# Reordering ScalarE's and VectorE's queues in a fused mLSTM and two-layer gated MLP kernel

## The chip, the core and the metric

One core of a Trainium2 chip runs the whole kernel in one launch. The metric is device time in microseconds of that core. The engines are TensorE (PE in the profile, its weight loads PEld), VectorE (DVE), ScalarE (ACT), GpSimd (POOL) and SyncE (SP), which here only issues DMAs. Each engine executes its own list of instructions in order; semaphores are the only link between them.

## The reference

```
for t in range(768):                       # B=2, H=8, D=40: a stabilised mLSTM
    m_new  = max(f[t] + m, i[t])
    C = exp(f[t]+m-m_new) * C + exp(i[t]-m_new) * outer(v[t], k[t])
    n = exp(f[t]+m-m_new) * n + exp(i[t]-m_new) * k[t]
    y[t] = sigmoid(o[t]) * (C @ q[t]) / max(|n . q[t]|, 1)
x = y as [1536 tokens, 320]
x = (sigmoid(x @ w_gate) * (x @ w_val)) @ w_out          # layer 1, d_ff = 1536
xn = x / rms(x) * rms_g                                  # layer 2
g = xn @ w_gate2;  out = (g * sigmoid(g) * (xn @ w_val2)) @ w_out2
```

All data are float32. The kernel computes each product of two float32 operands from rounded parts: a high part (`_hi`) and the remainder (`_lo`), three matmuls in place of one.

## The kernel before, in words

The 1536 tokens are 12 tiles of 128 (`NT`), numbered alternately over the two batches. The mLSTM is done by tiles; its pieces have one-letter names that every engine's `piece` function knows: D (decay weights by a matmul, then Exp on ACT), S (q·k scores on PE, sigmoid of the output gate on ACT), N, K, I (numerator, state update, state read), R (decays of a group of tiles: small PE matmuls, then two small Exp on ACT), Y (division on DVE), T (three PE transposes of a finished tile, ACT copies them to `x_hi`, DVE writes the remainder `x_lo`).

The first layer takes two phases. Tiles 0 to 7 go through it in four blocks of two tiles (`NB0`): a block is twelve slots `hidden(k, f)`, each of 16 matmuls for one 128-wide slice f of the gate and value products, followed by four halves of `project`, the down projection. The lists in `WEAVE` put the mLSTM pieces of later tiles between these slots, in the same order on all engines. Then come the wide blocks (`NB1`, four of them, k = 0 to 3): k = 0 is layer 1 for tiles 8 to 11, k = 1 to 3 are layer 2 for all twelve tiles, four tiles at a time.

In a wide block `hidden_pair(k, i)`, i = 0 to 5, computes slices f = 2i and 2i+1 in four phases: own half of slice f, own half of f+1, other half of f, other half of f+1. So slice f is finished (`g_done`, `v_done`) at the end of the third phase and slice f+1 at the end of the fourth. Behind each slice n runs a chain on two engines: `sigmoid(n)` on ACT (L620), `gate(n)` on DVE (L853; in layer 2 L851 ahead of it), `h_high(n)` on ACT (a Copy, L626), `h_low(n)` on DVE (L857), which counts up `h_done`. PSUM has eight banks, four in use by a pair and four by the pair before, so two places in PE's list wait for this chain:

```
if i > 1:
    pe.wait_ge(h_done, n - 3)                 # hidden_pair, phase of slice n
...
pe.wait_ge(h_done, n0 + NF - 2 if wide(n0) else ...)   # project, at each first half
```

The first asks for the same slice of the pair two before; the second asks for ten of the twelve slices of the block before the down projection starts; within the first token tile each further slice is waited for by itself.

The weights are loaded raw by SP into three rotating buffers, rounded by ACT in `high(layer, c)` (twelve chunks a layer; c below 8 are gate and value weights, L533), and the remainder is made by POOL in `split(layer, c)` (L435, L440), in order of c. `hidden(0, f)` waits at f = 0, 3, 6, 9 for two more splits each. SP reloads a raw buffer when its split is done.

At the start ACT's list is: D of tiles 0 and 1, `high(0,0)`, sigmoids S of tiles 0 and 1, `high(0,1)`, `high(0,2)`, the fill of `d_lhs` (L607), T(0), T(1), D(2), `high(0,3)`, D(3), R(1); then the slots. PE's is: T(0), idle matmuls, T(1), D(2), D(3), `hidden(0,0)`, R(1), `hidden(0,1)`. ACT holds one set of function tables; the compiler puts an ACT_TABLE_LOAD ahead of an Exp that follows a Sigmoid and ahead of a Sigmoid that follows an Exp. Copies run under either set.

Of the kernel before, what the change touches and what calls it, by code (L numbers as in the profile page):

```python
# [4 lines left out]
F32 = mybir.dt.float32  # L5
# [3 lines left out]
ACT = mybir.ActivationFunctionType  # L9
# [4 lines left out]
P = 128  # L14
# [8 lines left out]
NF = FF // P  # L23
# [15 lines left out]
F1 = NB0 * NF  # L39
# [33 lines left out]
def mlstm_moe_kernel(nc, gates, qk_t, vok, w_gv, w_o, rms_g, out):  # L73
# [5 lines left out]
    with ctx:  # L79
        def sb(name, shape, dt):  # L80
            return ctx.enter_context(nc.sbuf_tensor(name, shape, dt))
# [60 lines left out]
        meansq = sb("meansq", [P, B], F32)  # L142
        rstd = sb("rstd", [P, B], F32)
        half_neg = sb("half_neg", [P, 1], F32)
        eps = sb("eps", [P, 1], F32)


# [15 lines left out]
        def wide(n):  # L163
            return n >= F1
# [23 lines left out]
        def exp_base(n):  # L188

            return 0 if n == 3 else base(n)  # L190
# [18 lines left out]
        def raw_of(lay, c):  # L209
            r = (raw0, raw1)[lay][c % 3]  # L210
            if c < GVC:
                return r.rearrange("p (k c) -> p k c", k=3)
            return r[:, 0:FC * DM].rearrange("p (k c) -> p k c", k=FC)
# [34 lines left out]
        def part_of(j):  # L248
            return [j0 <= j < j1 for j0, j1 in PARTS].index(True)
# [272 lines left out]
        def _(act):  # L522
            def high(lay, c):
                whi = (whi0, whi1)[lay]
                if lay == 0:
                    act.wait_ge(raw0_in[c % len(raw0)], 16 * (c // len(raw0) + 1))
                else:
                    act.wait_ge(raw1_in[c % len(raw1)], 16 * (c // len(raw1) + 1))
                if c < GVC:
                    if lay == 1:  # L530
                        act.wait_ge(g_done, F1 + FC * (c // 2 + 1))
                        act.wait_ge(v_done, F1 + FC * (c // 2 + 1))
                    act.activation(wgv_hi[:, c, :, :], raw_of(lay, c), ACT.Copy).then_inc(whi, 1)  # L533
                else:
                    if lay == 1:
                        act.wait_ge(o_done, NT)
                    f0 = (c - GVC) * FC
                    act.activation(wo_hi[:, f0:f0 + FC, :], raw_of(lay, c), ACT.Copy).then_inc(whi, 1)

            def piece(what):  # L540
                kind, n, *_ = what
                b = n % B
                if kind == "D":
                    for i in range(2):
                        act.wait_ge(d_done, 2 * n + i + 1)
                        if n >= B and i == 0:
                            act.wait_ge(n_done, n - B + 1)
                        act.activation(wexp[b][:, 4 * i:4 * i + 4, :],
                                       bank[exp_base(n) + i][:, :].rearrange("p (q t) -> p q t", t=P),
                                       ACT.Exp).then_inc(e_done, 1)  # L550
                    if n < NT - B:

                        if n >= B:
                            act.wait_ge(vk_done, n - B + 1)
                        act.wait_ge(e_done, 2 * n + 2)
                        act.activation(el[:, b, :], wexp[b][:, :, P - 1], ACT.Copy).then_inc(el_done, 1)
                elif kind == "F":

                    act.wait_ge(rows_done, part_of(n) + 1)
                    act.wait_ge(fill_done, 2)  # L560
                    if n > 1:
                        act.wait_ge(d_done, 4 * n)
                    for w in range(2):
                        act.dma_start(d_rhs[R + w:R + w + 1, :, :].bitcast(F32),
                                      l_row[Q * w:Q * w + R, n % LR * P:(n % LR + 1) * P].bitcast(F32)).then_inc(flat_in, 16)
                elif kind == "R":
                    j0, j1 = PARTS[n]
                    act.wait_ge(r_mm, n)
                    act.activation(ecol[:, j0:j1, :], decay_t[:, j0:j1, :], ACT.Exp)
                    act.activation(gcol[:, j0:j1, :, :], decay_end[:, j0:j1, :, :], ACT.Exp).then_inc(r_exp, 1)  # L570
                elif kind == "S":
                    act.wait_ge(vo_in[b], 16 * (n // B + 1))
                    act.activation(o_sig[b], o_sig[b], ACT.Sigmoid).then_inc(osig_done, 1)
                elif kind == "T":
                    act.wait_ge(t_done, n + 1)
                    if n == 4:
                        act.wait_ge(split0, WCH)
                    if n == 8:
                        act.wait_ge(rows_done, len(PARTS))
                    act.activation(x_hi[:, n, :, :], t_view(bank[base(n) + 2]), ACT.Copy).then_inc(xh_done, 1)  # L580
                elif kind == "O":
                    act.wait_ge(ot_done, n + 1)
                    act.activation(x_hi[:, n, :, :], t_view(o_bank(n)), ACT.Copy).then_inc(xh2_done, 1)

            act.wait_ge(consts, 1)
            for b in range(B):
# [20 lines left out]
            act.activation(d_lhs[HALF:P, :, :, :], hide[HALF:P, :, :].unsqueeze(1).to_broadcast([HALF, NJ - 1, 2, P]),  # L607
                           ACT.Copy).then_inc(fill_done, 1)
            piece(("T", 0))
            piece(("T", 1))  # L610
            piece(("D", 2))
            high(0, 3)
            piece(("D", 3))
            piece(("R", 1))

            def sigmoid(n):
                act.wait_ge(g_done if wide(n) else v_done, n + 1)
# [4 lines left out]
            def h_high(n):  # L622
                act.wait_ge(hf_done, n + 1)
                if n % NF == 0 and n:
                    act.wait_ge(o_done, M0 + T1 * ((n - F1) // NF) if wide(n) else B * (n // NF))
                act.activation(h_view(n, 0), v_view(n), ACT.Copy).then_inc(hhi_done, 1)  # L626
# [21 lines left out]
            for k in range(NB1):  # L648
                for f in range(NF):
                    n = F1 + NF * k + f  # L650
                    sigmoid(n)
                    if f % 2:
                        h_high(n - 1)
                        h_high(n)
                    if k == 0 and f % FC == FC - 1:
                        high(1, 2 * (f // FC))
                        high(1, 2 * (f // FC) + 1)
                for t in range(T1):
                    m = M0 + T1 * k + t
                    if k == 0 and t < T1 - 1:  # L660
                        square(m)
                        piece(("O", M0 - B + t))
                        continue
                    if k == 0:
                        piece(("O", M0 - B + t))
                        square(m)
                        continue
                    act.wait_ge(o_done, m + 1)
                    if k == 1 and 0 < t <= B:
                        act.wait_ge(ot_done, NT - B + t)  # L670
                    if k > 1:
                        act.wait_ge(out_sent[t], 16 * (k - 1))
                    act.activation(y_out(t), o_view(m), ACT.Copy).then_inc(oe_done, 1)
                    if k == 1 and t < B:
                        piece(("O", NT - B + t))
                if k == 0:
                    for c in range(GVC, WCH):
                        high(1, c)
# [3 lines left out]
        def _(dve):  # L682
# [172 lines left out]
            def h_low(n):  # L855
                dve.wait_ge(hhi_done, n + 1)
                dve.tensor_tensor(h_view(n, 1), v_view(n), h_view(n, 0).bitcast(F32), ALU.subtract).then_inc(h_done, 1)  # L857
# [21 lines left out]
            for k in range(NB1):  # L879
                for f in range(NF):  # L880
                    n = F1 + NF * k + f
                    gate(n)
                    if f % 2:
                        h_low(n - 1)
                        h_low(n)
                if k == 0:
                    for t in range(T1):
                        piece(("O", M0 - B + t))
                        norm(M0 + t)
                elif k == 1:  # L890
                    for t in range(B):
                        piece(("O", NT - B + t))
# [3 lines left out]
        def _(pe):  # L896
# [242 lines left out]
            piece(("T", 1))  # L1139
            piece(("D", 2))  # L1140
            piece(("D", 3))
            hidden(0, 0)
            piece(("R", 1))
            for k in range(NB0):
                for slot in range(NF + 4):
                    if slot < NF:
                        if k or slot:
                            hidden(k, slot)
                    else:
                        t, half = divmod(slot - NF, 2)  # L1150
                        project(NF * k, B * k + t, t, half)
                    for what in WEAVE[k][slot]:
                        piece(what)
# [66 lines left out]
```

## Time and profile before

| | us |
|---|---|
| median of three runs (452.08 to 452.28) | 452.1 |
| the profiled execution's own time | 452.08 |
| its span, first to last instruction | 450.3 |
| PE busy | 444.9 (99%) |
| PEld busy | 404.2 (90%) |
| DVE busy | 211.3 (47%) |
| ACT busy | 186.8 (41%) |
| POOL busy | 97.0 (22%) |

Busy times are shares of the span. Matmuls overlap in the pipeline: a row of 128x512 in the wide blocks lasts 0.39 us while pairs of them start 0.23 us apart, so distances between starts, not durations, give TensorE's pace. In the timelines the first two columns are the start and the length in us; a bracket at the end holds the idle time of that engine ahead of the instruction, with what ended it.

### The profile page before, as it was taken

How to read it: one execution, taken by the hardware profiler on the slowest of the kernel's cores; microseconds unless marked ns; L12 is line 12 of the kernel's file. 1: busy time of each engine (PE TensorE's matmuls, PEld its weight loads, DVE VectorE, ACT ScalarE, POOL GpSimd, SP SyncE). 2: the span in 40 equal slices, each digit the busy share in tenths (PEclk: the TensorE clock that was granted, in tenths of full speed). 3: DMA queues.
4: the chain of work that ended last, by engine and by line, in shares of the span. 5: the costliest groups of instructions: out<-in, count | busy, mean ns of one | idle time of the engine just before them, and what ended most of it. 6: DMA issues, size and time to landing. Idle time of an engine off the chain costs nothing.

```text
span 450.3 us, 10548 instructions
## 1 busy us (share of the span) xinstructions
PE 444.9 (99%) x4489; PEld 404.2 (90%) x4489; DVE 211.3 (47%) x465; ACT 186.8 (41%) x355; POOL 97.0 (22%) x141
## 2 busy tenths in 40 slices
PE   8999999999999999999999999999999999999997
PEld 3799999999999999988889988889988899888897
DVE  8746746854476356424332217561055630256510
ACT  8976367554654463215544144231032320133310
POOL 2999711012101200013656172000000000000000
PEclk9999999999999999999999999999999999999999
DMA  7684600210221012100443110000000000000000
GB/s 253 208 264 136 206 3 1 77 62 17 75 75 58 22 45 90 70 1 2 121 132 102 44 45 1 1 0 31 31 2 0 1 16 29 16 1 2 0 31 29
DMA packets 10127, 25.91 MB, mean 58 GB/s; under 512 B 1376, under 2 KB 4480, under 8 KB 10080
## 3 DMA queue, kind: packets, MB, share of 16 engines
q1 hardware_dynamic: 9760, 25.15, 17.2%
q8 instruction: 35, 0.57, 0.5%
q10 hardware_dynamic: 320, 0.08, 0.1%
q14 instruction: 12, 0.10, 0.1%
HBM read 23.18 MB, written 1.97 MB: 56 GB/s over the span
## 4 chain that ended last, share of the span: by engine, by line
PE 95%; DVE 2%; POOL 2%; issue 0%; ACT 0%; POOLq 0%; DVEq 0%
PE bank L1097 36%; PE bank L1113 10%; PE bank L1115 9%; PE bank L1114 9%; PE bank L1046 8%; PE bank L1047 8%; PE bank L1049 5%; PE bank L965 2%; PE bank L996 2%; PE bank L899 2%; PE bank L984 1%; POOL wgv_lo L435 1%; PE bank L939 1%; PE bank L1005 1%; DVE first L832 1%; POOL wgv_hi L440 0%
## 5 line engine op out<-in xcount | busy, mean ns | idle before, releaser
L1097 PE MATMUL bank<-x_hi,wgv_hi 64*128 64x512 f32 x576 | 105.8, 388 | 0.0
L620 ACT ACTIVATE sg<-bank 128x256 f32<-128x256 f32 (+1 forms) x96 | 47.1, 492 | 131.0 <-PE bank L1097 82.3
L1097 PE MATMUL bank<-x_lo,wgv_hi 64*128 64x512 f32 x480 | 93.9, 386 | 0.0
L853 DVE TENSOR_TENSOR bank<-sg,bank 128x256 f32<-128x256 f32 (+1 forms) x96 | 53.8, 561 | 67.2 <-ACT sg L620 65.6
L1046 PE MATMUL bank<-x_hi,wgv_hi 128*128 128x256 f32 x288 | 80.5, 290 | 0.4 <-POOL wgv_hi L440 0.4
L1047 PE MATMUL bank<-x_lo,wgv_hi 128*128 128x256 f32 x288 | 78.3, 282 | 0.0
L1113 PE MATMUL bank<-wo_hi,h_hi 128*128 128x320 f32 x240 | 75.4, 314 | 0.0
L1097 PE MATMUL bank<-x_hi,wgv_lo 64*128 64x512 f32 x384 | 75.1, 386 | 0.0
L1115 PE MATMUL bank<-wo_hi,h_lo 128*128 128x320 f32 x240 | 74.1, 309 | 0.0
L1114 PE MATMUL bank<-wo_lo,h_hi 128*128 128x320 f32 x240 | 74.1, 309 | 0.0
L1097 PEld LDWEIGHTS bank<-x_hi,wgv_hi 64*128 64x128 f32 x576 | 54.4, 184 | 11.5 <-issue 0.7
L851 DVE TENSOR_TENSOR sg<-sg,bank 128x512 f32<-128x512 f32 x36 | 24.7, 687 | 83.0 <-ACT sg L620 83.0
L1046 PEld LDWEIGHTS bank<-x_hi,wgv_hi 128*128 128x128 f32 x288 | 55.0, 191 | 1.6 <-DVE x_lo L814 0.6
L1047 PEld LDWEIGHTS bank<-x_lo,wgv_hi 128*128 128x128 f32 x288 | 55.1, 191 | 0.0
L1049 PE MATMUL bank<-x_hi,wgv_lo 128*128 128x256 f32 x192 | 54.2, 283 | 0.0
L1097 PEld LDWEIGHTS bank<-x_lo,wgv_hi 64*128 64x128 f32 x480 | 45.4, 184 | 8.9
L1113 PEld LDWEIGHTS bank<-wo_hi,h_hi 128*128 128x128 f32 x240 | 45.1, 188 | 1.5 <-issue 1.4
L626 ACT ACTIVATE h_hi<-bank 128x256 fp32r<-128x256 f32 (+1 forms) x84 | 39.8, 474 | 15.0 <-DVE bank L853 15.0
L857 DVE TENSOR_TENSOR h_lo<-bank,h_hi 128x256 fp32r<-128x256 f32 (+1 forms) x84 | 44.8, 534 | 1.3
L1114 PEld LDWEIGHTS bank<-wo_lo,h_hi 128*128 128x128 f32 x240 | 45.1, 188 | 0.0
L1115 PEld LDWEIGHTS bank<-wo_hi,h_lo 128*128 128x128 f32 x240 | 45.1, 188 | 0.0
L1097 PEld LDWEIGHTS bank<-x_hi,wgv_lo 64*128 64x128 f32 x384 | 36.3, 184 | 7.3
(125 smaller groups left out, 546.8 us busy)
## 6 DMA issues: line engine op xcount, KB each, us to landing
step<-in_vok SPq DMA_DIRECT2D x12, 324.0 KB, 3.2
step<-in_qk_t SPq DMA_DIRECT2D x24, 160.0 KB
step<-in_w_gv SPq DMA_DIRECT2D x6, 576.0 KB, 3.9
raw_p<-in_w_gv SPq DMA_DIRECT2D x5, 576.0 KB, 3.9
raw_x<-in_w_gv SPq DMA_DIRECT2D x5, 576.0 KB, 5.0
step<-in_vok SPq DMA_DIRECT2D x10, 160.0 KB, 4.2
raw_x<-in_w_o SPq DMA_DIRECT2D x3, 480.0 KB, 3.5
raw_p<-in_w_o SPq DMA_DIRECT2D x3, 480.0 KB, 3.5
```

Source lines behind the costliest of these rows:

```text
L620: act.activation(sg_view(n), g_view(n), ACT.Sigmoid).then_inc(sg_done, 1)
L626: act.activation(h_view(n, 0), v_view(n), ACT.Copy).then_inc(hhi_done, 1)
L851: dve.tensor_tensor(sg_view(n), sg_view(n), g_view(n), ALU.mult).then_inc(silu_done, 1)
L853: dve.tensor_tensor(v_view(n), sg_view(n), v_view(n), ALU.mult).then_inc(hf_done, 1)
L857: dve.tensor_tensor(h_view(n, 1), v_view(n), h_view(n, 0).bitcast(F32), ALU.subtract).then_inc(h_done, 1)
L1046: pe.matmul(ps, wgv_hi[:, wc, s, cs], x_hi[:, xs, s, :], start=(s == 0), stop=False)
L1047: mm = pe.matmul(ps, wgv_hi[:, wc, s, cs], x_lo[:, xs, s, :], start=False, stop=(s == 2))
L1049: pe.matmul(ps, wgv_lo[:, wc, s, cs], x_hi[:, xs, s, :], start=False, stop=False)
L1097: mm = pe.matmul(ps(n), w, x, start=own and (s, p) == (0, 0), stop=last and not own)
L1113: pe.matmul(ps, h_view(n0 + f, 0)[:, ts], wo_hi[:, f, :], start=(f == 0), stop=False)
L1114: pe.matmul(ps, h_view(n0 + f, 0)[:, ts], wo_lo[:, f, :], start=False, stop=False)
L1115: mm = pe.matmul(ps, h_view(n0 + f, 1)[:, ts], wo_hi[:, f, :], start=False, stop=(f == NF - 1))
```

## The change

Four edits. (1) A one-column Exp into a new tile `spare` is put on ACT between T(0) and T(1). (2) `high(0,3)` goes from between D(2) and D(3) to behind R(1) on ACT. (3) On PE `hidden(0,0)` goes behind R(1). (4) In the wide blocks, `h_high(n-1)` on ACT and `h_low(n-1)` on DVE follow `sigmoid(n)` and `gate(n)` for every n, instead of two of them after every odd n; the last slice's follow the loop, on ACT in block k = 0 behind `high(1,6)` and `high(1,7)`.

```diff
+        spare = sb("spare", [P, 1], F32)
...
             piece(("T", 0))
+
+            act.activation(spare[:, :], half_neg[:, :], ACT.Exp)
             piece(("T", 1))
             piece(("D", 2))
-            high(0, 3)
             piece(("D", 3))
             piece(("R", 1))
+            high(0, 3)
...  (ScalarE, wide blocks)
                     sigmoid(n)
-                    if f % 2:
+                    if f:
                         h_high(n - 1)
-                        h_high(n)
                     if k == 0 and f % FC == FC - 1:
                         high(1, 2 * (f // FC))
                         high(1, 2 * (f // FC) + 1)
+                h_high(F1 + NF * k + NF - 1)
...  (VectorE, wide blocks)
                     gate(n)
-                    if f % 2:
+                    if f:
                         h_low(n - 1)
-                        h_low(n)
+                h_low(F1 + NF * k + NF - 1)
...  (TensorE, start)
             piece(("D", 3))
-            hidden(0, 0)
             piece(("R", 1))
             for k in range(NB0):
                 for slot in range(NF + 4):
                     if slot < NF:
-                        if k or slot:
-                            hidden(k, slot)
+                        hidden(k, slot)
```

## Rows read from the trace of the kernel before

**Rows 1.** The chain that ended last, by engine, from the page.
```profile
PE 95%; DVE 2%; POOL 2%; issue 0%; ACT 0%; POOLq 0%; DVEq 0%
```
**Rows 2.** Windows of wide block k=1: length, busy by engine, granted clock, DMA.
```profile
260.00:323.00 63.00, 63.00 (x512) 55.41 (x512) 26.45 (x41) 20.34 (x37) 11.15 (x14) 1.00 0.05 17
```
**Rows 3.** Timeline of PE, from D(3)'s matmuls to slot 3.
```profile
18.41 1.20 PE L939 MATMUL bank<-d_rhs,d_lhs 128*128 128x256 f32 x8
20.02 0.35 PE L1046 MATMUL bank<-x_hi,wgv_hi 128*128 128x256 f32 x1 [0.42 <-POOL wgv_hi L440]
...
21.89 0.28 PE L1047 MATMUL bank<-x_lo,wgv_hi 128*128 128x256 f32 x1
...
22.47 0.39 PE L1046 MATMUL bank<-x_hi,wgv_hi 128*128 128x256 f32 x1
22.70 0.28 PE L1047 MATMUL bank<-x_lo,wgv_hi 128*128 128x256 f32 x1
...
27.62 0.28 PE L1046 MATMUL bank<-x_hi,wgv_hi 128*128 128x256 f32 x1
```
**Rows 4.** Timeline of ACT from T(1) to R(1).
```profile
18.68 0.49 ACT L580 ACTIVATE x_hi<-bank 128x384 fp32r<-128x384 f32 x1 [0.39 <-PE bank L899]
19.20 1.28 ACT L548 ACT_TABLE_LOAD   x1
20.49 1.09 ACT L548 ACTIVATE tail<-bank 128x512 f32<-128x512 f32 x2
...
21.80 1.15 ACT L533 ACTIVATE wgv_hi<-raw_p 128x1152 fp32r<-128x1152 f32 x1
...
24.19 0.17 ACT L570 ACTIVATE gcol<-bank 128x8 f32<-128x8 f32 x1
```
**Rows 5.** Timeline of all engines, the DVE row of T(1).
```profile
19.21 0.56 DVE L814 TENSOR_TENSOR x_lo<-bank,x_hi 128x384 fp32r<-128x384 f32 x1 [0.32 <-ACT x_hi L580]
```
**Rows 6.** Timeline of POOL, the ends of split(0,1) and split(0,3).
```profile
18.87 1.00 POOL L440 TENSOR_TENSOR wgv_hi<-raw_x,wgv_hi 64x384 fp32r<-64x384 f32 x1
...
25.16 0.99 POOL L440 TENSOR_TENSOR wgv_hi<-raw_p,wgv_hi 64x384 fp32r<-64x384 f32 x1
```
**Rows 7.** Timeline of ACT, end of wide block k=0.
```profile
239.14 2.21 ACT L533 ACTIVATE wgv_hi<-step 128x1152 fp32r<-128x1152 f32 x2
```
**Rows 8.** Timeline of DVE, end of wide block k=0: gate(10).
```profile
236.32 0.70 DVE L853 TENSOR_TENSOR bank<-sg,bank 128x512 f32<-128x512 f32 x1 [2.15 <-ACT sg L620]
```
**Rows 9.** Timeline of PE, block k=0: first matmul of project, and its slice 10.
```profile
237.14 0.41 PE L1113 MATMUL bank<-wo_hi,h_hi 128*128 128x320 f32 x1
...
241.64 0.31 PE L1113 MATMUL bank<-wo_hi,d_rhs 128*128 128x320 f32 x1
```
**Rows 10.** Timeline of ACT, wide block k=1, slices 8 to 10.
```profile
292.53 0.60 ACT L620 ACTIVATE sg<-bank 128x512 f32<-128x512 f32 x1 [2.53 <-PE bank L1097]
...
294.61 0.60 ACT L626 ACTIVATE h_hi<-bank 128x512 fp32r<-128x512 f32 x1
...
299.33 0.60 ACT L620 ACTIVATE sg<-bank 128x512 f32<-128x512 f32 x1 [2.53 <-PE bank L1097]
```
**Rows 11.** Timeline of DVE, wide block k=1, slices 8 to 10.
```profile
295.47 0.69 DVE L853 TENSOR_TENSOR bank<-sg,bank 128x512 f32<-128x512 f32 x1
296.07 0.68 DVE L857 TENSOR_TENSOR h_lo<-bank,h_hi 128x512 fp32r<-128x512 f32 x1
...
299.96 0.69 DVE L851 TENSOR_TENSOR sg<-sg,bank 128x512 f32<-128x512 f32 x1 [2.44 <-ACT sg L620]
300.68 0.70 DVE L853 TENSOR_TENSOR bank<-sg,bank 128x512 f32<-128x512 f32 x1
```
**Rows 12.** Timeline of PE, the first matmul of project in block k=1.
```profile
300.77 0.41 PE L1113 MATMUL bank<-wo_hi,h_hi 128*128 128x320 f32 x1
```
**Rows 13.** Timeline of PE, idle matmuls at the start and later.
```profile
1.26 6.22 PE L1125 MATMUL bank<-inter 128*128 128x512 bf16 x21 [1.26 <-DVE inter L821]
...
15.70 1.04 PE L1125 MATMUL bank<-inter 128*128 128x512 bf16 x4
```

## The prediction, made before the changed kernel ran

> **What bounds the kernel now.** I read the chain of waits first. Nearly all of the chain that ended last is TensorE [rows 1], and in a window over a wide block TensorE is busy for all of its 63.00 us at a granted clock of 1.00 [rows 2]. So there is nothing later in the run that could take up a delay: whatever holds TensorE back at one place is added to the end, and whatever lets it start earlier is taken off. The other engines matter only where TensorE waits for them, or comes close to it. I then read the timelines of each engine around the four edits: 16 to 28 us for the first three, and the end of each wide block for the fourth.
>
> **Edits 1 and 3, the start.** TensorE ends D(3) at 18.41 + 1.20 = 19.61 and starts `hidden(0,0)` at 20.02 [rows 3]. It waits for two things that come close together: the second split, 18.87 + 1.00 = 19.87 [rows 6], and the remainder of tile 1, 19.21 + 0.56 = 19.77 [rows 5]. The idle 0.42 us is put down to the first, but the second has only 0.10 us of room.
>
> What edit 3 takes away: R(1) and the two switches around it. `hidden(0,0)` starts its last matmul at 21.89, and `hidden(0,1)` its second at 22.70 [rows 3]. Sixteen matmuls from 20.02 to 21.89 are 0.12 apart (1.87 / 15 = 0.125, with a longer first step). Without R(1) in between, the second of the next slot would start two steps after 21.89, at 22.13. That is 0.57 earlier. R(1) itself fits in the idle time: with its switches it takes under 22.47 - 21.89 = 0.58 [rows 3], and the gap is at least 0.41 and, as follows, becomes longer. It waits for nothing late: its inputs, the row ends on VectorE, are made before the scores of tiles 0 and 1.
>
> What edit 1 adds: ScalarE ran out of work at 18.68 - 0.39 = 18.29, then waited for T(1)'s transposes, copied them to 18.68 + 0.49 = 19.17, and only then loaded the Exp tables, 1.28 us [rows 4]. With the small Exp behind T(0) the load starts at 18.32, ends at 19.60, the Exp follows at 19.61 (the next activation starts 0.01 after a load: 19.20 + 1.28 to 20.49 [rows 4]) and takes 0.17 at most, a little less until the next one starts; I take 0.15. The copy of T(1) then starts at 19.76, not 18.68: 1.08 late. Only 0.39 us of the load is hidden in ScalarE's idle time, and the rest is put in front of a copy that TensorE needs. Its end moves to 20.25, the remainder's end on VectorE from 19.77 to 20.85, and `hidden(0,0)` starts some 0.05 later, at 20.90: 0.88 late. Edits 1 and 3 together: +0.88 - 0.57 = +0.31 us. From both sides: if the table load did not hold up the copy behind it, T(1) would be as early as now and the start would gain the whole 0.57; if R(1) filled nothing and the small Exp cost its full 0.17, the loss would be 0.90. I take +0.3, since the load's row leaves ScalarE no room for another instruction.
>
> The row has the load at 1.28 us and the Exp 0.01 behind it [rows 4]. The Trainium skill ("ScalarE: Activation LUTs", section "What ACT_TABLE_LOAD costs") gives a switch of sets 1.28 us and a drain of 1.38 beside it, 2.66 together. By that rule the copy of T(1) would be another 1.38 late and the start would cost +1.7, not +0.3. The row shows no such drain on either side of the load, so the trace does not agree here, and the sum goes by the row.
>
> **Edit 2, the first weights.** ScalarE is done with D(2), D(3) and R(1) sooner: `high(0,3)` was in between, from 21.80 for 1.15 [rows 4]. Now T(1)'s copy ends at 20.25 and D(2)'s Exps follow without a load, 0.3 earlier than 20.49. D(3) and R(1) then end at 24.36 - 1.15 - 0.3 = 22.9, and `high(0,3)` ends near 24.0 instead of 22.95. POOL's split(0,3) ended at 25.16 + 0.99 = 26.15 [rows 6] and now ends at about 27.2. TensorE asks for it in slot 3, at 27.62, now 27.9 [rows 3]. Room is left, 0.7 us, so it costs nothing. If ScalarE or POOL slipped by more than that, each further microsecond would be one for TensorE; the same delay, reduced by a short idle of POOL, goes through the later splits and raw loads, where slots 6 and 9 have more room than slot 3. I take 0, with 0 to +0.7.
>
> **Edit 4, the wide blocks.** This is the costly one. Now slice 9, the second of pair 4, is finished on the other engines right after pair 4, 6.8 us ahead of its use. In the new order `h_high(9)` stands behind `sigmoid(10)`, and `h_low(9)` behind `gate(10)`. Slice 10 is finished by TensorE only at the end of the third phase of pair 5; a single phase later TensorE reaches `project` and asks for ten slices, slice 9 among them.
>
> Block k = 1: `sigmoid(10)` starts at 299.33 [rows 10], L851 at 299.96 and L853 at 300.68 [rows 11]. The L857 behind an L853 starts 0.60 after it (295.47 to 296.07) and lasts 0.68 to 0.69. So `h_low(9)` runs from 301.28 to 301.97. `h_high(9)`, 0.60 long [rows 10], is done by 300.53 and is not in the way. TensorE's `project` begins at 300.77 now [rows 12] and at 301.97 + 0.05 = 302.02 then: a stall of 1.25 us. Blocks 2 and 3 have the same instructions at the same distances, so 3 x 1.25 = 3.75.
>
> Block k = 0 has no L851. `gate(10)` starts at 236.32 [rows 8], `h_low(9)` at 236.92, ending at 237.61; `project` moves from 237.14 [rows 9] to 237.66: 0.52 us.
>
> Is there a second loss inside the blocks? Phase two of pair i waits for the odd slice of pair i - 2, which now hangs on the even slice of pair i - 1. In k = 1 that is slice 7 behind slice 8: `sigmoid(8)` at 292.53 [rows 10], and the chain takes 301.97 - 299.33 = 2.64, so 295.17. TensorE starts the second phase of pair 5 later than that: pair 5 begins about when slice 9 is done, 1.6 us (a phase of 14 steps at 0.23 for two) behind slice 8, and its first phase of 16 matmuls lasts 1.8, so near 295.8. Room 0.6: nothing lost. In k = 0, `high(1,6)` and `high(1,7)`, 2.21 us for both [rows 7], now stand ahead of `h_high(11)`. `h_high(10)` starts near 237.8, the two run from 238.3 to 240.5, `h_high(11)` to 241.0, `h_low(11)` to 241.75. TensorE needs slice 11 one slice (three matmuls, 0.44) behind 241.64 [rows 9], plus the stall of 0.52, near 242.6. Room 0.8: nothing. If the raw chunk for `high(1,7)` came late, that room would be used first.
>
> **The sum.** +0.3 (start) + 0 (edit 2) + 0.52 (k = 0) + 3.75 (k = 1 to 3) = +4.6 us. The profiled execution took 452.08, which is the median of the runs within 0.02, so 456.7; I say 456.6, as the small Exp may overlap more.
>
> **The rivals.**
> (a) The covers of 0.6 to 0.8 us above are too thin: a split at slot 3, `h_low(7)` in the second phase, or `h_high(11)` is late. For it: three such places, each with under 1 us. Against it: all three are computed from rows that repeat within 0.01. It would give +0.5 to +1.5 more, about 457.7.
> (b) The clock falls in the new idle stretches ahead of `project`. At the start of the run, after an idle stretch of 1.26, TensorE needed 6.22 us for 21 matmuls of a kind that later run 1.04 for four, 0.22 apart; that is some 1.5 us more than 20 x 0.22 + 0.38 = 4.8 [rows 13]. If it fell in all three stretches of 1.25 us: +4.5 more, 461. Against it: the clock held 1.00 over idle 0.42 [rows 3], and the gaps stay short beside the busy time around them. The rule in the Trainium skill ("TensorE: Matmul & The Clock Gate", section "Part 1: The HAM clock gate") that an idle array falls back to 1.2 GHz speaks for it in kind.
> (c) Not slower: `h_done` of slice 9 comes before TensorE asks. That would need the chain sigmoid, gate, h_low behind slice 10 to be shorter than 300.77 - 299.33 = 1.44 us in k = 1, where the rows give 2.64; from that point on the stall is nothing, and only the start is left, +0.3 or, with the table load hidden too, -0.57. It would give 451.5 to 452.4, say 452.3. It could be so only if VectorE or ScalarE ran another order than the diff says.
>
> **How the numbers follow.** Forecast 0.82, (a) 0.09, (b) 0.05, (c) 0.04. The forecast's own range is from the start's bound without the late copy (-0.57, so 455.8) to 457.2. The range for 8 in 10 reaches some way to (a): 455.6 to 457.9. A difference of 0.2%, 0.9 us, is about what can be told from no change; slower by more than that holds for the forecast, (a) and (b), 0.95; (c) is within it, 0.04; faster 0.01.
>
> **What would show it.** The profile after should have four idle stretches of PE ahead of the down projection (L1113), 0.5 us once and 1.25 three times, released by VectorE's L857; `hidden(0,0)` starting at 20.9, released by VectorE's L814, with `hidden(0,1)` right behind; ACT_TABLE_LOAD at 18.3; no PE idle in slots 3 to 9 or in the second phases; clock 1.00. The forecast is wrong if the stretches ahead of L1113 are missing, or if PE idles anywhere else by more than 0.3 us.

## The result and the profile after

The changed kernel takes 456.8 us (median of four runs, 456.64 to 457.32) against 452.09: 4.7 us or 1.05% more, ratio 1.0105, interval 1.0088 to 1.0122. The forecast was 456.6 in 455.6 to 457.9. The profiled execution took 456.61 with a span of 454.8, 4.5 longer than before.

The page after, its busy times by engine, the granted clock and the chain by engine:

```profile
PE 445.1 (98%) x4489; PEld 404.1 (89%) x4489; DVE 208.1 (46%) x465; ACT 184.3 (41%) x356; POOL 96.5 (21%) x141
...
PEclk9999999999999999999999999999999999999999
...
PE 93%; DVE 3%; ACT 3%; issue 1%; ACTq 0%; DVEq 0%
```

TensorE works as long as before (445.1 against 444.9); the 4.5 us are time in which it waits. Where it waits, the groups of its instructions with the idle time ahead of them show at once (name, count, busy us and mean ns, idle us and releaser):

```profile
L1049 PE MATMUL bank<-x_hi,wgv_hi 128*128 128x256 f32 x288 | 80.4, 290 | 0.8 <-DVE x_lo L817 0.8
...
L1116 PE MATMUL bank<-wo_hi,h_hi 128*128 128x320 f32 x240 | 75.4, 314 | 4.0 <-DVE more_lo L860 4.0
```

The first is the start, the second the four first matmuls of `project`. L1116 and L860 are the L1113 and L857 of before. No other group waits more than it did. The same four places in the timeline of PEld, whose idle time also holds the switch between two kinds of matmul. Before, the rows at these places all read 0.35:

```profile
237.94 0.19 PEld L1116 LDWEIGHTS bank<-wo_hi,h_hi 128*128 128x128 f32 x1 [0.88 <-DVE more_lo L860]
...
302.82 0.19 PEld L1116 LDWEIGHTS bank<-wo_hi,h_hi 128*128 128x128 f32 x1 [1.60 <-DVE more_lo L860]
...
367.06 0.19 PEld L1116 LDWEIGHTS bank<-wo_hi,h_hi 128*128 128x128 f32 x1 [1.60 <-DVE more_lo L860]
...
430.64 0.19 PEld L1116 LDWEIGHTS bank<-wo_hi,h_hi 128*128 128x128 f32 x1 [1.59 <-DVE more_lo L860]
```

0.88 - 0.35 = 0.53, then 1.25, 1.25, 1.24: together 4.27. What stands behind them in block k = 1 is this piece of VectorE's timeline, to be laid beside [rows 11]:

```profile
300.75 0.69 DVE L854 TENSOR_TENSOR sg<-sg,bank 128x512 f32<-128x512 f32 x1 [2.87 <-ACT sg L623]
301.47 0.69 DVE L856 TENSOR_TENSOR bank<-sg,bank 128x512 f32<-128x512 f32 x1
302.08 0.68 DVE L860 TENSOR_TENSOR more_lo<-bank,d_rhs 128x512 fp32r<-128x512 f32 x1
```

The L860 at 302.08 is `h_low(9)`. It ends at 302.76, and TensorE starts at 302.82. VectorE had been idle for 2.87 us ahead of `gate(10)`, and ScalarE for 4.12 us ahead of `sigmoid(10)`: between them they had had the time to do `h_high(9)` and `h_low(9)`, but the order of both lists forbade it.

The start, TensorE's timeline first (to be read beside [rows 3]), then ScalarE's (beside [rows 4]):

```profile
18.41 1.19 PE L942 MATMUL bank<-d_rhs,d_lhs 128*128 128x256 f32 x8
19.53 0.23 PE L950 MATMUL bank<-ident,l_r 16*128 16x16 f32 x1
19.69 0.28 PE L953 MATMUL bank<-l_end,ones 16*64 16x8 f32 x4
20.82 0.38 PE L1049 MATMUL bank<-x_hi,wgv_hi 128*128 128x256 f32 x1 [0.84 <-DVE x_lo L817]
```

```profile
17.79 0.49 ACT L581 ACTIVATE x_hi<-bank 128x384 fp32r<-128x384 f32 x1
18.30 1.28 ACT L612 ACT_TABLE_LOAD   x1
19.60 0.20 ACT L612 ACTIVATE spare<-half_neg 128x1 f32<-128x1 f32 x1
19.71 0.47 ACT L581 ACTIVATE x_hi<-bank 128x384 fp32r<-128x384 f32 x1
```

R(1) is in the gap, the table load is in front of T(1)'s copy, and `hidden(0,0)` starts at 20.82, 0.80 late. Slot 3 starts at 27.89 against 27.62: 0.27 late, the shift that the start leaves. 4.27 + 0.27 = 4.54 is the whole of the 4.5.

### The profile page after: what moved, and what is told of

Its sections match the earlier page's. It is cut to its first block, busy times and chain, and to the rows that moved or that the text cites. A ratio compares the mean times of both kernels' runs of the same rounds, so it can differ in the third digit from the quotient of the medians.

```text
span 454.8 us, 10549 instructions
## 1 busy us (share of the span) xinstructions
PE 445.1 (98%) x4489; PEld 404.1 (89%) x4489; DVE 208.1 (46%) x465; ACT 184.3 (41%) x356; POOL 96.5 (21%) x141
## 4 chain that ended last, share of the span: by engine, by line
PE 93%; DVE 3%; ACT 3%; issue 1%; ACTq 0%; DVEq 0%
PE bank L1100 35%; PE bank L1116 10%; PE bank L1118 9%; PE bank L1117 9%; PE bank L1049 8%; PE bank L1050 8%; PE bank L1052 5%; PE bank L968 2%; PE bank L999 2%; PE bank L902 2%; PE bank L987 1%; PE bank L942 1%; PE bank L1008 1%; ACT wgv_hi L534 1%; DVE more_lo L860 1%
## 5 line engine op out<-in xcount | busy, mean ns | idle before, releaser
L1116 PE MATMUL bank<-wo_hi,h_hi 128*128 128x320 f32 x240 | 75.4, 314 | 4.0 <-DVE more_lo L860 4.0
L854 DVE TENSOR_TENSOR sg<-sg,bank 128x512 f32<-128x512 f32 x36 | 24.6, 683 | 88.7 <-ACT sg L623 88.7
L1116 PEld LDWEIGHTS bank<-wo_hi,h_hi 128*128 128x128 f32 x240 | 45.1, 188 | 5.8 <-DVE more_lo L860 5.7
L860 DVE TENSOR_TENSOR h_lo<-bank,h_hi 128x256 fp32r<-128x256 f32 (+1 forms) x84 | 44.6, 531 | 0.2
```

Of the source, the lines that this page charges most:

```text
L854: dve.tensor_tensor(sg_view(n), sg_view(n), g_view(n), ALU.mult).then_inc(silu_done, 1)
L1116: pe.matmul(ps, h_view(n0 + f, 0)[:, ts], wo_hi[:, f, :], start=(f == 0), stop=False)
```

## Experiments

Each time is a median over the runs of a comparison in which the kernel before took 452.08 to 452.11.

**order_only**, edit 4 alone: the two `if f % 2` loops replaced as in the change, nothing at the start.

> Edit 4 alone, on the kernel before. Theory (slice 9's h_low behind gate(10) makes TensorE wait ahead of project): idle 0.5 + 1.25 + 1.25 + 1.25 us of PE ahead of project and nowhere else, time 452.1 + 4.25 = 456.35. Rival (the loss needs the later start, or the start carries more than 0.3): under 455.5.

456.39 us (456.36 to 456.43), ratio 1.0094 (1.0080 to 1.0108). PE's idle time ahead of L1113 is 4.0 us in four places, as in the changed kernel. Edit 4 costs 4.3.

**start_only**, edits 1 to 3 alone.

> Edits 1 to 3 alone, wide blocks as before. Theory: hidden(0,0) 0.8 late, R(1) in the gap takes 0.57 off, so 452.1 + 0.3 = 452.4, and no PE idle after slot 0. Rival (the late weights of edit 2 cost something): over 452.8.

452.43 us (452.36 to 453.02), ratio 1.0009 (1.0000 to 1.0018): +0.34. The profiled execution, one of the slower ones (452.85), has no idle row of PE after the start. Together with order_only that is 4.6, against 4.7 for the whole change. The parts add up.

**pe_swap**, edit 3 alone.

```diff
-            hidden(0, 0)
             piece(("R", 1))
...
-                        if k or slot:
-                            hidden(k, slot)
+                        hidden(k, slot)
```

> Edit 3 alone: hidden(0,0) behind R(1) on TensorE, ScalarE's list as before. Theory: R(1) lies wholly in the idle time ahead of hidden(0,0), which still starts at 20.02; the time falls by 0.57 to 451.5. Rival (R(1) pushes hidden(0,0) back by its own length): 452.1, no change.

451.63 us (451.53 to 451.88), ratio 0.9990 (0.9981 to 0.9999): -0.47. In TensorE's timeline R(1) starts at 19.75 and `hidden(0,0)` at 20.13 with no idle time between:

```profile
18.64 1.19 PE L939 MATMUL bank<-d_rhs,d_lhs 128*128 128x256 f32 x8
19.75 0.23 PE L947 MATMUL bank<-ident,l_r 16*128 16x16 f32 x1
19.91 0.28 PE L950 MATMUL bank<-l_end,ones 16*64 16x8 f32 x4
20.13 0.39 PE L1046 MATMUL bank<-x_hi,wgv_hi 128*128 128x256 f32 x1
```

R(1) takes 0.38 with its switch and pushes `hidden(0,0)` back by 0.1 in this execution, in which D(2) was late as well (D(3)'s row starts at 18.64, not 18.41). The fastest of the eleven took 451.53, the time that the theory gives, and the rival's 452.1 is out. This is the only version here that is faster than before, by 0.1%, with an interval that just leaves out 1.

**warm_only**, edit 1 alone, the line with `act.activation(spare, ..., ACT.Exp)`.

> Edit 1 alone: the one-column Exp between T(0) and T(1). Theory: only the 0.4 us of ScalarE's idle time hide the table load, the copy of T(1) and so hidden(0,0) come 0.8 later: 452.9. Rival (the load runs beside the copy of T(1)): 452.1. With a drain of 1.38 us beside the load, as the Trainium skill, page ScalarE: Activation LUTs, section What ACT_TABLE_LOAD costs, has it, 454.3.

453.10 us (452.93 to 454.40), ratio 1.0026 (1.0015 to 1.0037): +1.0, where 0.8 was expected. In the profiled execution (452.96) `hidden(0,0)` starts at 20.84, 0.82 late, and PE idles 1.23 ahead of it, released by the DVE row of T(1); the rest of the 1.0 is the spread of the seven. The load is not beside the copy. A drain is not seen either: the median is 1.2 below 454.3, and in the rows of the changed kernel above the Exp follows the load's end (19.58) by 0.02. One of the seven took 454.40, but at a granted clock of 0.996, where the other six have 1.000; the last section comes back to it.

**nine_early**, the changed kernel with slice 9 alone in the old order.

```diff
-                    if f:
+                    if f and f != 10:
                         h_high(n - 1)
+                    if f == 9:
+                        h_high(n)
...  (and the same with h_low on VectorE)
```

> The changed kernel, but slice 9 of each wide block as before: h_high(9) and h_low(9) directly behind slice 9's own sigmoid and gate, all other slices in the new order. Theory (only slice 9 is late for TensorE): all four stalls vanish, 452.4, as edits 1 to 3 alone. Rival (the new order costs in the inner pairs or at slices 10 and 11 too): over 453.

452.44 us (452.36 to 453.93), ratio 1.0011 (1.0002 to 1.0020): start_only's time. All four rows of PEld ahead of `project` are back at 0.35. One of twelve slices in each block carried the 4.3 us; the new order of the others costs nothing that can be seen.

**dve_order** and **act_order**, edit 4 on one engine only.

> The new order on VectorE alone, ScalarE's as before. Theory: h_low(9) waits for VectorE's own gate(10), and that alone sets the stall, 0.5 + 3 x 1.25: 456.35. Rival (ScalarE's late h_high(9) is part of it): clearly less.

> The new order on ScalarE alone, VectorE's as before. Counted from sigmoid(10)'s start: h_high(9) ends at 0.50 + 0.60 = 1.10, h_low(9) runs 1.13 to 1.82, project could start at 1.87 in place of 1.44. Theory: 0.43 us in each of the four blocks, the same in layer 1 and layer 2, since gate(10) now stands behind h_low(9): 452.1 + 1.7 = 453.8. Rival (ScalarE's order costs nothing by itself): 452.1.

dve_order: 456.68 us (456.61 to 456.89), ratio 1.0101 (1.0087 to 1.0115). act_order: 453.75 us (453.75 to 453.95), ratio 1.0036 (1.0024 to 1.0049). PEld ahead of `project` in block k = 1, first dve_order, then act_order:

```profile
302.82 0.19 PEld L1113 LDWEIGHTS bank<-wo_hi,h_hi 128*128 128x128 f32 x1 [1.60 <-DVE more_lo L857]
```

```profile
301.61 0.19 PEld L1113 LDWEIGHTS bank<-wo_hi,h_hi 128*128 128x128 f32 x1 [0.77 <-DVE more_lo L857]
```

VectorE's order alone makes the full stall; ScalarE's alone 0.77 - 0.35 = 0.42 in every block, since there `h_low(9)` stands ahead of `gate(10)` and waits for `h_high(9)`. The two do not add: the late `h_high(9)` is hidden behind the later `h_low(9)`. dve_order is 0.3 above order_only. A further stall that I had not expected holds most of it, one wait in block k = 1, in the phase that asks for slice 1:

```profile
275.92 0.19 PEld L1097 LDWEIGHTS bank<-x_hi,wgv_hi 64*128 64x128 f32 x2 [0.33 <-DVE h_lo L857]
```

ScalarE's list is held at the head of that block by `high(1,11)`, whose raw chunk lands late (4.44 us of idle time ahead of it), so `sigmoid(0)` begins only at 269.35 and the first slices come in a queue. What ScalarE's old order adds is that `h_high(1)` stands ahead of `sigmoid(2)`, which starts at 273.23 here and at 272.65 in order_only; `gate(2)` and, behind it in VectorE's new order, `h_low(1)` come later by as much. The room of 0.6 us that the prediction computed for the inner pairs from slices 7 and 8 is not there for slice 1. In the changed kernel this place holds with some 0.3 us: `h_low(1)` ends at 275.56.

**no_silu**, the changed kernel without L854, layer 2's product of sigmoid and gate.

> The changed kernel without layer 2's multiplication of the sigmoid by the gate (L854 in it), which leaves that factor out of the result. Theory (the stall is the length of the chain behind slice 10): blocks 1 to 3 stall 0.53 like block 0, 456.7 - 3 x 0.72 = 454.5. Rival (the stall is a fixed cost of the new order, in ScalarE or TensorE): 456.7.

454.52 us (454.48 to 455.12), ratio 1.0056 (1.0042 to 1.0070). The rows ahead of `project` are 0.88, 0.88, 0.88 and 0.87: a stall of 0.53 in each block. One instruction of 0.72 us from start to start taken out of the chain behind slice 10 takes 0.72 off each of three stalls.

**swap_high** and **late_high**, edit 2 with edit 3, and edit 2 alone; neither has the early Exp. In both, `high(0,3)` goes behind D(3) and R(1).

> Edits 2 and 3 without the early Exp and without the new order of the wide blocks. Theory: edit 3's 0.5 us stays, edit 2 costs nothing beside it: 451.6. Rival (edit 2 is felt): over 451.9.

> Edit 2 alone, no early Exp, R(1) behind hidden(0,0) as before. In the kernel with edits 2 and 3 split(0,3) ended at 27.56 and TensorE idled 0.39 ahead of slot 3. Here slot 3 comes 0.57 later than in that kernel would be its turn, at 27.62. Theory (the room at slot 3 is a difference of two clocks, ScalarE's and TensorE's): almost no idle at slot 3, under 0.15, and only what the later waits for split(0,11) and for D(4)'s rows take: 452.1 to 452.5. Rival (edit 2 has its own cost wherever slot 3 stands): 453.1, one more than before, as swap_high is one more than pe_swap.

swap_high: 452.71 us (452.36 to 453.11), ratio 1.0013 (1.0004 to 1.0022). late_high: 452.57 us (452.31 to 453.21), ratio 1.0009 (1.0000 to 1.0018). The theory for swap_high fails, and late_high lies just above its theory's span (452.1 to 452.5) and 0.5 below the rival's 453.1. Edit 2 is not free: by the medians it costs 1.1 on top of edit 3 and 0.5 alone, by the fastest executions 0.83 and 0.26. The difference is what the theory expects, but the intervals of the four medians together are about as wide as it, so that the cost depends on where slot 3 stands rests more on the rows than on the times. In swap_high the two ends of the room meet at slot 3, in PE's timeline and POOL's:

```profile
27.62 0.39 PE L1046 MATMUL bank<-x_hi,wgv_hi 128*128 128x256 f32 x1 [0.39 <-POOL wgv_hi L440]
```

```profile
24.51 1.98 POOL L435 TENSOR_TENSOR wgv_lo<-raw_p,wgv_hi 128x384 fp32r<-128x384 f32 x2 [1.46 <-ACT wgv_hi L533]
26.56 1.00 POOL L440 TENSOR_TENSOR wgv_hi<-raw_p,wgv_hi 64x384 fp32r<-64x384 f32 x1
```

The row of PE shows 0.39 of the wait; by the starts, slot 3 comes 0.66 later than in pe_swap. In late_high's profile slot 3 waits as well, which the theory put under 0.15: its first weight load starts at 28.09, 0.26 later than the start of `hidden(0,0)` explains. A second place shows there, in block 0's `project`: slice 9 of the first tile waits for the last of the first layer's splits.

```profile
55.76 0.39 PE L1113 MATMUL bank<-wo_hi,h_hi 128*128 128x320 f32 x1 [0.33 <-POOL wo_lo L449]
```

In swap_high the same place costs 0.2, by the starts. The profiled execution of late_high is the slowest of its eleven (453.21): ScalarE's list ran 0.8 us late from the start on (the fill of `d_lhs` ended at 18.55, not 17.79), so it does not say what edit 2 alone costs in a fast one (452.31). The spread differs too: the kernel before stays within 0.3 us over its fifteen runs beside it, the kernels with edit 1 or edit 2 cover 0.5 to 0.9 (leaving out two executions with a granted clock of 0.996), pe_swap, without either, 0.35.

**pushed**, edits 1 to 3 with 1.6 us of other work ahead of `high(0,3)`.

```diff
             piece(("R", 1))
+            for t in range(2):
+                act.activation(filler[:, t * 768:(t + 1) * 768], half_neg[:, :].to_broadcast([P, 768]), ACT.Copy)
             high(0, 3)
```

> Edits 1 to 3 alone, plus two Copies of 768 columns into an unused tile on ScalarE ahead of high(0,3), 0.8 us each, 1.6 together. Theory: split(0,3) ended at 27.13 in the changed kernel's profile and slot 3 asks for it at 27.89, so 0.7 of the delay is covered and TensorE idles 0.9 in slot 3: 452.4 + 0.9 = 453.3. Rival (edit 2 has far more room than computed): 452.4. Rival (later slots have less room than slot 3): over 453.6.

454.02 us (453.39 to 454.19), ratio 1.0039 (1.0026 to 1.0051): 1.6 above start_only, the whole of the added work. Half of it is at slot 3, as the theory has it (28.66 against 27.89 in the changed kernel: 0.8), the rest further on, in PE's timeline:

```profile
28.66 0.39 PE L1053 MATMUL bank<-x_hi,wgv_hi 128*128 128x256 f32 x1 [0.60 <-POOL wgv_hi L443]
...
66.05 0.71 PE L946 MATMUL bank<-d_rhs,d_lhs 128*128 128x256 f32 x4 [0.43 <-DMA d_rhs<-l_row]
```

The rival "later slots have less room" holds in the time; the place is not a slot but D(4). It waits for two small DMAs (a piece named F(2)) that ScalarE issues after VectorE has made the rows. Those rows stand in VectorE's list behind gates that wait for sigmoids, and the sigmoids behind the `high` copies of late raw chunks (one such copy waits 2.89 us for its chunk and starts at 51.52; in the kernel before it waits 1.35 and starts at 47.89). In the kernel before F(2) was issued from 58.84 on, in this one from 61.75 on.

## Why the prediction was right, and where a step was off

- **Edit 4** carried the loss as computed: 0.52 and 3 x 1.25 forecast, 0.53, 1.25, 1.25 and 1.24 measured. order_only shows that it is this edit, nine_early that it is slice 9 and nothing else, no_silu that the price follows the length of the chain (one link of 0.72 was varied), and dve_order and act_order which engine's order sets it.
- **Edit 1** was sized at 0.88 late and came 0.80 late: the one-column Exp costs 0.11 to the next start, not 0.15, and VectorE's row starts 0.50 behind the start of the copy (19.71 to 20.21), not 0.53. TensorE follows that row's end by 0.05, as forecast. **Edit 3** took 0.53 off instead of 0.57 (0.80 - 0.27).
- **The drain beside the table load**, which the prediction names from the Trainium skill ("ScalarE: Activation LUTs", section "What ACT_TABLE_LOAD costs"), would have made the start +1.7. The trace does not agree: start_only measured +0.34, and the load has neighbours at 0.02 us on both sides.
- **Edit 2** was priced at 0 in the changed kernel, which holds (PE has no idle in slots 1 to 11), but that it holds leans on edit 1, which the prediction did not say. The step put the room at slot 3 at 0.7 us, which measured 0.76 (27.13 to 27.89), and gave the later slots more. The room at slot 3 is the difference of ScalarE's and TensorE's times, and edit 1 helps it on both sides: it ends ScalarE's work 0.4 earlier and starts TensorE's 0.8 later. Without edit 1 there is none: swap_high waits there. And two places that I had not named, the last split in block 0's `project` and F(2)'s DMAs for D(4), take part when the delay is larger. In single parts, medians: edit 1 +1.0, edit 2 +0.5, edit 3 -0.5; all three +0.34. They do not add: on top of edits 2 and 3 (swap_high, +0.6) edit 1 does not cost 1.0. It costs nothing that can be seen (452.43 against 452.71, with intervals that overlap, and 452.36 for the fastest execution of both).
- **The second loss inside the blocks** was excluded with a room of 0.6 us taken from slices 7 and 8. True for the changed kernel, but dve_order shows a thinner place at slice 1 of block k = 1.
- **The rivals**: (b) did not happen ahead of `project`, where the granted clock reads 1.00 across idle stretches of 1.25 us. Its price of 1.5 us was read from one execution's first matmuls, whose slow part varies (last section). (c) did not happen; (a) had the right kind of place and did not come into play.
- **Left open**: why the changed kernel's median lies 0.2 above its profiled run, which was its fastest. start_only, with the same start, has a profile of a slower execution (452.85, 0.5 above its fastest), and there `hidden(0,0)` starts at 21.23, 0.41 later than in the changed kernel's profile. The same would explain the 0.2, but no slower execution of the changed kernel was profiled.

## What to carry to other kernels

When an in-order engine is told to finish a piece of work "one step later", look for the consumer with the least room, not for the average: work that is ready and has an idle engine in front of it still waits if it is queued behind something that is not ready, and the price is the length of the whole chain behind the late input less the room the consumer had. Work out each cover from both of its ends and follow the queue to its last consumer. Edits that move both ends of one room cannot be priced one by one.

## What was not expected of the hardware

Between executions ScalarE's first 17 us vary: `high(0,0)` started at 11.09, 11.08, 11.48 and 11.86 in the profiles of the kernel before, the changed one, start_only and late_high, whose lists are the same up to there. The delay comes from TensorE. ScalarE waits for the first product of D(0), and TensorE makes it behind its first 21 idle matmuls, which took 6.22 us before [rows 13], 7.28 in start_only and 7.66 in late_high. Late_high's rows, of PE and of ACT:

```profile
1.26 7.66 PE L1125 MATMUL bank<-inter 128*128 128x512 bf16 x21 [1.26 <-DVE inter L821]
```

```profile
9.40 1.08 ACT L548 ACTIVATE tail<-bank 128x512 f32<-128x512 f32 x2 [1.02 <-PE bank L934]
```

In the kernel before that idle time of ScalarE is 0.25. The weight loads of these matmuls start 0.43 us apart at first and 0.22 later, and the change comes at 4.2 us in the kernel before, at 6.4 in start_only and at 7.2 in late_high. A pace that doubles speaks for TensorE's clock, but the granted clock reads 1.00 in the profiles there too, so that is not shown, and why it comes later in some executions stays open.

Which kernel feels it depends on its rooms. dve_order has the start of the kernel before, and with `high(0,0)` at 11.50 its `hidden(0,0)` still starts at 20.05, against 20.02: the delay is absorbed. In start_only the same delay of 0.4 is one of 0.41 for `hidden(0,0)`.

The two longest outliers are something else. One execution of warm_only (454.40) and one of nine_early (453.93) lie 1.5 us above the fastest of their kernel and are the only ones with a granted clock of 0.996; all others have 0.999 or 1.000. Of their span of 452 us, 0.4% is 1.8 us, an estimate of the size of the loss. Both kernels have the early Exp and with it the longer idle time of TensorE ahead of `hidden(0,0)`; neither execution was profiled, so where the clock fell is not shown.
